# A fused attention and two-stage expert kernel: the end of attention and the first expert tiles in another order

## The reference

```python
# 1. gated linear attention, B=4, H=8, S=768, D=48
f = 1 / (1 + exp(-f_logit))
state = f[t] * state + outer(k[t], v[t]);  y[t] = q[t] @ state
# 2. top-1 experts: 3072 tokens, width 384, 8 experts, hidden 1024
logits = x @ w_gate + modality_bias[modality_id]
e = argmax(logits);  gate = softmax(logits)[e]      # denominator + 1e-9
x = gate * (relu(x @ w1[e]) @ w2[e])
# 3. gated MLP, hidden 1536
xn = x / sqrt(mean(x * x) + 1e-6) * rms_g
g = xn @ w_gate2
out = (g * sigmoid(g) * (xn @ w_val)) @ w_out
```

## Time and profile before

| | |
|---|---|
| median of 3 runs (lowest to highest) | 866.95 us (866.81 to 869.07) |
| profiled execution | 866.84 us, span 865.1 us |
| granted TensorE clock, mean | 0.988 |
| TensorE busy | 833.0 us, 96% |
| TensorE weight load | 762.5 us, 88% |
| VectorE busy | 471.8 us, 55% |
| ScalarE busy | 389.6 us, 45% |
| GpSimd busy | 165.6 us, 19% |
| DMA | 96.49 MB, mean 112 GB/s |

### The profile page before, as it was taken

The page is one execution under the profiler, slowest core; times in us unless marked ns, Lnnn a source line. Parts: engine busy times, 40 slices in busy tenths (PEclk is TensorE's granted clock), DMA queues, the critical chain, the costliest instruction groups (busy, mean ns, idle before and its releaser), DMA issues.

```text
span 865.1 us, 15457 instructions
## 1 busy us (share of the span) xinstructions
PE 833.0 (96%) x5332; PEld 762.5 (88%) x5332; DVE 471.8 (55%) x773; ACT 389.6 (45%) x750; POOL 165.6 (19%) x165
## 2 busy tenths in 40 slices
PE   6999999779999999989999999999999999999997
PEld 6798988779999999989888888888888898888887
DVE  7989898687766666653444333334333333433332
ACT  5988786375666555653423411331241133123112
POOL 5444352318554000000000200100020010001001
PEclk9999999889999999999999999999999999999999
DMA  9877666497988797750200200100020000000000
GB/s 182 188 148 169 150 146 210 153 387 239 301 258 260 245 344 255 255 147 20 74 1 1 74 0 1 66 8 0 0 73 0 0 28 8 0 0 36 0 0 36
DMA packets 44082, 96.49 MB, mean 112 GB/s; under 512 B 9168, under 2 KB 25040, under 8 KB 43920
## 3 DMA queue, kind: packets, MB, share of 16 engines
q1 hardware_dynamic: 39952, 85.81, 33.6%
q0 software_dynamic: 3840, 9.47, 3.1%
q10 hardware_dynamic: 256, 0.79, 0.4%
HBM read 76.75 MB, written 19.29 MB: 111 GB/s over the span
## 4 chain that ended last, share of the span: by engine, by line
PE 78%; issue 2%; DVE 1%; POOL 0%; ACT 0%; DVEq 0%; ACTq 0%
PE h_ps L1779 16%; PE h_ps L1781 15%; PE h_ps L1780 15%; PE ym_ps L1779 7%; PE ym_ps L1781 7%; PE ym_ps L1780 7%; PE xTm_ps L1780 3%; PE xTm_ps L1779 3%; PE xTm_ps L1781 3%; PE xT_ps L1796 1%; PE xTm_ps L1787 1%; POOL out L1443 0%; DVE h_lo L1691 0%; DVE w_lo L1664 0%; ACT w_hi L1461 0%
## 5 line engine op out<-in xcount | busy, mean ns | idle before, releaser
L1754 DVE TENSOR_TENSOR gs<-h_ps,sig 128x512 f32<-128x512 f32 x72 | 49.8, 691 | 175.5 <-ACT sig L1555 175.5
L1555 ACT ACTIVATE sig<-h_ps 128x512 f32<-128x512 f32 x72 | 43.1, 598 | 158.9 <-PE h_ps L1781 158.9
L1566 ACT CAST h_hi<-hid 128x512 fp32r<-128x512 f32 x72 | 44.6, 620 | 150.2 <-DVE hid L1757 150.2
L1779 PE MATMUL h_ps<-x_hi,w_hi 128*128 128x256 f32 x312 | 89.7, 287 | 7.7 <-DVEq L1682 5.1
L1781 PE MATMUL h_ps<-x_lo,w_hi 128*128 128x256 f32 x312 | 89.3, 286 | 0.0
L1780 PE MATMUL h_ps<-x_hi,w_lo 128*128 128x256 f32 x312 | 89.1, 285 | 0.0
L1779 PE MATMUL h_ps<-w_hi,wg_hi 128*128 128x512 f32 x216 | 85.5, 396 | 0.0
L1781 PE MATMUL h_ps<-w_lo,wg_hi 128*128 128x512 f32 x216 | 84.6, 392 | 0.0
L1781 PE MATMUL h_ps<-w_lo,wv_hi 128*128 128x512 f32 x216 | 84.2, 390 | 0.0
L1780 PE MATMUL h_ps<-w_hi,wv_lo 128*128 128x512 f32 x216 | 84.0, 389 | 0.0
L1779 PE MATMUL h_ps<-w_hi,wv_hi 128*128 128x512 f32 x216 | 84.0, 389 | 0.0
(11 more groups left out here) (222 smaller groups left out, 1890.0 us busy)
## 6 DMA issues: line engine op xcount, KB each, us to landing
w_raw<-in_w SPq DMA_DIRECT2D x52, 384.0 KB, 5.0
w_in<-in_w SPq DMA_DIRECT2D x52, 384.0 KB, 5.1
qkf_in<-in_qkf SPq DMA_DIRECT2D x43, 288.0 KB, 5.0
y_sorted<-x_group SPq DMA_DIRECT2D x13, 384.0 KB, 3.4
v_in<-in_v SPq DMA_DIRECT2D x24, 192.0 KB, 4.3
x_regions<-zero_row SPq DMA_DIRECT2D x12, 384.0 KB, 2.9
x_group<-x_regions SPq DMA_DIRECT2D x12, 384.0 KB, 3.9
g_in<-in_wg SPq DMA_DIRECT2D x3, 768.0 KB, 8.1
```

What stands on the lines that cost most here:

```text
L1555: nc.scalar.activation(sig[:], g_ps, ACT.Sigmoid).then_inc(sig_done, 1)
L1566: nc.scalar.copy(h2_hi[:, fb % HELD], hid[:]).then_inc(h2_hi_done, 1)
L1754: nc.vector.tensor_tensor(gs[:], g_ps, sig[:], ALU.mult).then_inc(gs_done, 1)
L1779: nc.tensor.matmul(out, hi, rhs_hi, start=first, stop=False)
```

## The change

It reorders; no arithmetic is added or left out.

1. Drain of attention: SP issues the weights of the first expert ahead of the last two v loads. Tile 23's keys are no longer transposed and copied (its state update is not used), and its read goes into the bank `ks_ps`, one phase earlier on TensorE, behind it the flag matmul and then the product of tile 22. ScalarE casts w1 quarters 0, 1, 2, 3 and copies in a new order. VectorE's flag steps, `lo_w1(2)` and `lo_x` move ahead of the logits of their step; `lo_w1(3)` moves into `experts`.
2. `experts`, tile 0: SP raises its semaphores ahead of three DMA issues, w2 first. ScalarE casts all four quarters of w2 at once. VectorE does `lo_w1(3)` behind `choose`. TensorE's count stands in the middle of hidden(0). `shifted_scores`, `rows_of_tokens`, `gates_of_tokens`, the Exp, the table load and thirds 0 and 1 leave the tile; `rows_of_tiles` goes to VectorE's end of it; `lo_w2(0, 3)` behind `lo_h(2)`. SP waits for rows_ready only before the store of y in tile 1.
3. Ends of middle tiles: VectorE does `shifted_scores` in tile 1, `rows_of_tokens` in tile 2, `gates_of_tokens` in tile 3. ScalarE casts third i in tile i + 1 (0 to 5 in tiles 1 to 6), with the Exp in tile 2. SP loads thirds 3 to 5 in tiles 3 to 5, `wo` in tile 8. POOL issues the token scatters eight at a time behind thirds 3, 4 and 5.
4. Last tile: ScalarE does `hi_h(0)` before the squares, and loads the sigmoid table behind `hi_h(1)`.

The diff, cut to its core:

```diff
@@ SP, attention
-            for b in range(2):
-                load_v(*tile(CH, b, 2))
-
             sp.wait_ge(ahead_sems.picked, PICKS)
             e = first.expert_of(sp)
             first.load_weights(sp, e, w1, w2, ahead_sems)
+            for b in range(2):
+                load_v(*tile(CH, b, 2))
@@ ScalarE, attention
-                if t := tile(c, b, 1):
+                if (t := tile(c, b, 1)) and not at(c, CH):
...
+                if at(c, CH) and b == 1:
+                    first.hi_w1(nc, act, 3, ahead_sems)
+                    kept(tile(c, b, 2), ks_ps)
...
                 if at(c, CH) and b == 0:
-                    first.hi_w1(nc, act, 1, ahead_sems)
+                    for g in range(2):
+                        first.hi_w1(nc, act, g, ahead_sems)
+                if (t := tile(c, b, 2)) and not (at(c, CH) and b == 1):
+                    kept(t, yT_ps)
+                if at(c, CH) and b == 0:
+                    first.hi_w1(nc, act, 2, ahead_sems)
...
+            def kept(t, acc):
+                _, s, n = t
+                act.wait_ge(y_done, n + 1)
+                wait_past(act, x_done, n - 1)
+                nc.scalar.copy(yT[:, s % 2], acc[:]).then_inc(yT_kept, 1)
@@ VectorE, attention
-                if at(c, CH) and b == 2:
+                if at(c, CH) and b == 1:
+                    first.lo_w1(nc, dve, 2, ahead_sems)
                     dve.wait_ge(flag_sum, 1)
...
+                if at(c, CH) and b == 2:
+                    first.lo_x(nc, dve, xT_ps, ahead_sems)
...
-                if at(c, CH) and b == 1:
-                    first.lo_w1(nc, dve, 2, ahead_sems)
-                if at(c, CH) and b == 2:
-                    first.lo_x(nc, dve, xT_ps, ahead_sems)
-                    first.lo_w1(nc, dve, 3, ahead_sems)
@@ TensorE, attention (read() is the old code of tile(c, b, 2))
-                    wait_past(pe, ks_done, n)
-                    for j in range(PR):
-                        mm = nc.tensor.transpose(ks_ps[:, j], kT[:, s, j], ident[:])
-                    mm.then_inc(k_turned, 1)
+                    if not at(c, CH):
+                        wait_past(pe, ks_done, n)
+                        for j in range(PR):
+                            mm = nc.tensor.transpose(ks_ps[:, j], kT[:, s, j], ident[:])
+                        mm.then_inc(k_turned, 1)
...
+                if at(c, CH) and b == 1:
+                    pe.wait_ge(ks_done, NT - 1)
+                    read(c, b, tile(c, b, 2), ks_ps)
+                    pe.wait_ge(small_ready, 1)
+                    nc.tensor.matmul(flag_ps, rt.ones_r[:], small[:], start=True, stop=True).then_inc(flag_sum, 1)
@@ experts
-        WO_AT = 7
+        WO_AT = 8
@@ SP, experts
+            sp.sem_inc(y_stored, 16)
+            sp.sem_inc(x_landed, 16)
+            for g in range(GR):
+                sp.sem_inc(w2_landed[g], 16)
+                sp.sem_inc(w1_landed[g], 16)
             for i in range(EARLY):
                 load_third(i)
...
                     load_third(EARLY)
-                    sp.wait_ge(rows_ready, 1)
...
                 if place == "middle":
+                    sp.wait_ge(rows_ready, 1)
                     store_y(j - 1)
...
-                            with only(sp, j, i - KD + 1):
+                            with only(sp, j, i):
                                 load_third(i)
@@ POOL, experts
-            pool.wait_ge(pos_ready, 1)
-            pool.wait_ge(gate_ready, 1)
...
-                for n in range(i * (NT // 6), (i + 1) * (NT // 6)):
+                if i == KD:
+                    pool.wait_ge(pos_ready, 1)
+                    pool.wait_ge(gate_ready, 1)
+                for n in range(max(i - KD, 0) * (NT // KD), max(i - KD + 1, 0) * (NT // KD)):
@@ ScalarE, experts
-            hi_w2(0, 0)
+            for g in range(GR):
+                hi_w2(0, g)
...
+                hi_h(0)
+                if place != "first":
+                    next_w1(0)
                 if place == "last":
                     act.wait_ge(norm_in, 16)
                     square(0, 0)
-                hi_h(0)
-                if place == "first":
-                    hi_w2(0, 1)
-                else:
-                    next_w1(0)
                 hi_h(1)
-                if place == "first":
-                    hi_w2(0, 2)
-                    act.wait_ge(shifted, 1)
-                    nc.scalar.activation(prob, biased, ACT.Exp).then_inc(exp_ready, 1)
+                if place == "last":
                     nc.scalar.preload_act_table_set("sigmoid_and_others")
-                    hi_w2(0, 3)
...
-                    hi_third(0)
...
-                if place == "first":
-                    hi_third(1)
                 if place == "middle":
-                    with act.If(j < 2 * KD):
-                        for i in range(EARLY, 2 * KD):
-                            with only(act, j, i - 1):
+                    with act.If(j < 2 * KD + 1):
+                        for i in range(2 * KD):
+                            with only(act, j, i + 1):
                                 hi_third(i)
+                                if i == 1:
+                                    act.wait_ge(shifted, 1)
+                                    nc.scalar.activation(prob, biased, ACT.Exp).then_inc(exp_ready, 1)
@@ VectorE, experts
-            dve.sem_inc(w1_split, GR)
+            dve.sem_inc(w1_split, GR - 1)
             dve.sem_inc(x_split, 1)
             rt.choose(nc, dve, CH - 1, marks, 0)
+            lo_w1(0, GR - 1)
             lo_w2(0, 0)
...
                     lo_w2(0, 1)
-                    shifted_scores()
                     lo_w2(0, 2)
-                    lo_w2(0, 3)
-                    rows_of_tiles()
...
                 lo_h(2)
                 if place == "first":
+                    lo_w2(0, 3)
...
                 if place == "first":
-                    rows_of_tokens()
-                    gates_of_tokens()
+                    rows_of_tiles()
+                if place == "middle":
+                    with dve.If(j < 4):
+                        with only(dve, j, 1):
+                            shifted_scores()
+                        with only(dve, j, 2):
+                            rows_of_tokens()
+                        with only(dve, j, 3):
+                            gates_of_tokens()
@@ TensorE, experts
                     for i in range(2):
+                        if place == "first" and g == 0 and i == 1:
+                            pe.wait_ge(marks, Routing.CHOSEN)
+                            rt.count(nc, pre_ps, cnt_ps).then_inc(counted, 1)
...
                 hidden(0)
-                if place == "first":
-                    pe.wait_ge(marks, Routing.CHOSEN)
-                    rt.count(nc, pre_ps, cnt_ps).then_inc(counted, 1)
                 hidden(1)
```

More of the change, by code:

```diff
@@ L722, in growth, with read @@
                 mm.then_inc(ds_done, 1)
+            def read(c, b, t, acc):
+                cc, s, n = t
+                if not tile(c, b, 1):
+                    pe.wait_ge(masked, n + 1)
+                if at(c, 0):
+                    pe.wait_ge(consts, CONSTS)
+                pe.wait_ge(v_landed[s], (cc + 1) * 16)
+                if not at(c, CH) and not (at(c, 0) and b == 2):
+                    growth(s, n)
+                wait_past(pe, state_done, n - 3)
+                if not at(cc, 0):
+                    for j in range(PR):
+                        nc.tensor.matmul(acc[:, j], state[:, s, j], qT[:, s, j], start=(j == 0), stop=False,
+                                         skip_group_check=True)
+                if at(cc, 0):
+                    pe.wait_ge(yT_zero, 1)
+                for j in range(PR):
+                    for par in range(2):
+                        h, r = 2 * j + par, PAD * par
+                        mm = nc.tensor.matmul(acc[r:r + D, j], v_in[:, s, D * h:D * (h + 1)],
+                                              scores[:, s % 2, par, j], start=at(cc, 0), stop=(at(cc, 0) or j == PR - 1),
+                                              skip_group_check=True)
+                mm.then_inc(y_done, 1)
             def step(c, b, half, more):
@@ L751, in step @@
                     mm.then_inc(x_done, 1)
[L752 to L772, removed]
-                            mm = nc.tensor.matmul(yT_ps[r:r + D, j], v_in[:, s, D * h:D * (h + 1)],
-                                                  scores[:, s % 2, par, j], start=at(cc, 0), stop=(at(cc, 0) or j == PR - 1),
-                                                  skip_group_check=True)
-                    mm.then_inc(y_done, 1)
+                if (t := tile(c, b, 2)) and not (at(c, CH) and b == 1):
+                    read(c, b, t, yT_ps)
                 if b == B - 1 and not (at(c, 0) or at(c, CH)):
@@ L782, in step @@
                 if at(c, CH) and b == 1:
-                    pe.wait_ge(small_ready, 1)
```

(8 more changed lines are left out.)

12 lines of the change are left out of this document (2 added, 10 removed).

## The result

The kernel after took 878.93 us (median of 4, 876.52 to 883.37) beside 868.01 of the kernel before (now the median of 4, the three of the table above and one of 873.08): a ratio of 1.012 with a 95% interval of 1.0062 to 1.0178. The forecast of 863.2 and its range up to 871.3 were both missed. The profiled execution took 878.87 us (span 877.1), 12.0 more than that of before.

What follows compares the result with a forecast made beforehand. TensorE, 96% busy, was taken as the bound, with some 13 us to be had at most. From 866.84 us, -6.95 - 0.32 + 0.3 + 3.3 = -3.65 gave 863.2 us, range 860 to 871.3.

Steps and rivals of the forecast that it cites:

- Into the experts, -0.75: Between attention and first expert tile: dropped transposes let POOL finish earlier, so TensorE starts at 159.55, 0.75 us sooner.
- Tile 0: First expert tile: table 1.05 us earlier, the 1.83 us wait goes, new wait about 2.4, clock +0.3 (0 to 0.65).
- Tile 1: Second expert tile: wait 1.3 instead of 3.17, half clock and 1.49 wait go; tile 2 starts at 202.3, -6.95 us.
- The ends of the tiles, +3.3: Ends of tiles 1, 2, 3: VectorE's moved chains make TensorE wait 0.9, 2.1 and 0.3 us, together +3.3 (1.8 to 12).
- 0.58 per chain: Ends of tiles 1 to 3: extra delay per chain beside POOL's subtractions, 0.73 - 0.15 us, from small ops.
- The row of 0.19: At 115.69 in the trace before: a small op inside a POOL operation of 1.51 us took its usual 0.19 us.
- The rival of the port: Ends of tiles 1 and 2: POOL's subtractions hold small VectorE ops, waits 3.3 and 5.1 us; 869.8 us, 27%.
- Eight token scatters per third instead of four: Middle tiles, POOL: the larger groups take some 10 us of a 17.67 us tile, cost nothing, covered by idle time.
- The last tile, -0.32: Last expert tile: squares follow h_hi(0), so the 0.32 us TensorE wait goes.
- chains hide entirely: Ends of tiles 1 to 3: rival in which the moved VectorE chains cost TensorE nothing; 861 us, 5%.
- one chain caught: End of tile 2: rival in which only its chain, longest under POOL, is held; +3 over forecast, 866.3 us, 15%.
- data bound: Tiles 0 and 1: rival in which data of tiles 1 and 2 land no earlier, the table's lead worthless; 865.5 us, 8%.

Runs made afterwards that it cites:

- b_scatter8: Kernel before with its token scatters grouped eight at a time behind thirds 3 to 5, nothing else touched: 873.89 us, ratio 1.005.
- the first trace: First profiled execution of the kernel after, unchanged: 878.87 us; median of that run 878.93 us, ratio 1.012.
- the first and the last experiments: First: four variants of the kernels, 869.29 to 875.69 us. Last, on a fourth chip: kernel after unchanged 881.07 us, and with a wait before each fourth scatter 871.25 us.
- b_scatter8_2: Kernel before with scatters in groups of eight, run again on a third chip: 866.99 us, ratio 0.9994.
- a_best_x: Version with both repairs, but SyncE loads tile 1's rows after the second instead of the fourth piece of w1: 863.59 us, ratio 0.995.
- a_best_x3: Version with both repairs, but SyncE loads tile 1's rows after the third instead of the fourth piece of w1: 863.01 us, ratio 0.9948.
- the version with both repairs: Kernel after with VectorE's chains in mid tile and scatters four at a time in tiles 5 to 10: 862.15 us (0.9941), repeated 864.27 us (0.9965).
- a_scatter4: Kernel after with its 24 token scatters four at a time over tiles 5 to 10, not eight over tiles 5 to 7: 873.01 us, ratio 1.0052.
- the first four experiments: Kernel after with scatters in fours, chains mid tile, or third casts later; kernel before with scatters in eights: ratios 1.0052, 1.0009, 1.0082, 1.005.
- after_fifth: Kernel after, unchanged, run again on a fourth chip: 881.07 us (two executions), ratio 1.0145.
- the third trace: Profiled execution of the kernel after, unchanged, run a third time, on a third chip: 869.79 us, ratio 1.0034.

## Why the prediction was wrong, point by point

- **Into the experts, -0.75: right in size, invisible in the time.** From the scores of the last but one step to the first expert matmul it was 160.30 - 142.08 = 18.22 us before and 160.31 - 142.70 = 17.61 after, 0.61 less; it is 17.60 to 17.69 in every trace with the new order, and 18.21 and 18.61 in the two of b_scatter8. All of it was lost in attention itself, whose end moves from run to run: in two traces of b_scatter8 the first expert matmul is at 158.80 and at 163.27.

```profile
142.70 1.22 DVE L631 TENSOR_TENSOR scores<-sc_ps,tri 128x1024 f32<-128x1024 f32 x1
```

- **Tile 0: the mechanism right, the clock too small.** The table was ready 9.66 us after the first expert matmul (169.97; forecast 9.75), and the rows were waited for 2.95 us (2.4). The clock behind that wait was counted at +0.3, up to 0.65. It was 0.66 in that stretch, and gather_y(3) with 12 matmuls took 185.46 - 181.73 = 3.73 us where a steady one takes 2.08: 1.6 us. Tile 1 started 25.15 us after the first expert matmul instead of 23.75.
- **Tile 1: right.** 18.67 us against 19.0, with a wait of 0.80 where 1.3 was forecast.
- **The ends of the tiles, +3.3: the step that failed.** Tile 1's chain cost 0.9, as said, tile 3's nothing, but tile 2's 7.2 instead of 2.1. The price of 0.58 per chain was taken from "a small op inside a POOL operation took 0.19" and another of 0.73, because they were nearest in size. Size did not spare them: operations that take 0.24 us alone took 1.36 and 1.20. The row of 0.19 was no measure of that, for it lies beside another form of GpSimd operation, with one source in place of two, and starts only 0.28 us before that ends. And the row of 0.73 (128.94 to 129.67) was a hold itself: a GpSimd operation that the forecast did not look up ends at 129.70. The two splits that were held lay beside the same subtractions as the new chains, and were the rows to take. The rival of the port priced tile 2's wait at 5.1 and had the sum at 869.8; where there was no stall, the kernel after measured 869.8 to 871.5. The cause is the rival's, but that its sum fits is in part luck: it had tile 1's chain at 3.3, which cost 0.9, while the gain up to tile 2 that it started from was 1.5 us too large. The mechanism differs in one point: three small operations were let in one by one, each as a subtraction ended, where the rival had the first held until the third ended. That is why tile 1's chain, of which a single operation was caught (1.39 us at 207.22), stayed cheap.

In the kernel before, GpSimd beside the earlier trace rows:

```profile
128.64 1.06 POOL L137 DMA_INDIRECT x_regions<-x_group,row  x1 [8.69 <-DVE row L132]
```

So the 0.58 was, as these rows have it, not the price of any collision but the rest of one GpSimd operation of 1.06; with three subtractions of 1.25 in a row the same reading gives three times up to 1.25. Which pairs of operations collide the runs show only in part: `chosen<-biased,first` (128x32, two sources, at 116.83) took 0.22 in the midst of a GpSimd DMA_INDIRECT of 1.06 (116.35).

- The Trainium skill's rule on this ("SBUF — State Buffer", section "SBUF: two separate sides"), that the shared pair of ports is locked for a whole instruction, agrees with the trace: 1.36, 1.20 and 1.36 us against subtractions of 1.25, and 0.24, 0.24 and 0.36 when GpSimd was away. The forecast set the row of 0.19 against it and left the rival at 27%; it deserved the larger share. What the runs show is the hold beside GpSimd's subtractions; that a port makes it is the page's account.
- **"Eight token scatters per third instead of four take some 10 us of a tile of 17.67; ... nothing, covered by idle time": the second step that failed.** GpSimd did have the time. What was not costed is what eight in a row do outside GpSimd: 7.2 us in tile 6 and 0.7 in tile 8, in the first trace, the like on the chips of the first and the last experiments, and nothing on the two others. No row of before showed more than four in a row, so the cost had no bound from above, and the forecast gave it none. Why the core stalls behind them stays open.
- **The last tile, -0.32:** 32.76 against 33.32 where the clock stayed up, -0.56. In the first trace the clock was 0.66 at its start and the tile 0.9 longer than before; the kernel before can have it too, for b_scatter8_2, whose last tile is the kernel before's, took 34.24.
- The rival "chains hide entirely" fell, and "one chain caught" had the right chain at 3 us over the forecast where it was 5.1; "data bound" did not decide the change, but it stopped a_best_x and a_best_x3.

## What to carry to other kernels

Work moved into idle time of one engine has to be asked twice: which engine shares a port with it there, and how many transfers it has under way. Price a collision from rows with the same neighbour, not from rows of the same size; and where a change raises a count above any that the trace shows, such as scatters in a row, give it an upper bound or spread it. The same change, with its chains some 7 us earlier and its scatters in fours, is 0.3 to 0.6% faster than the kernel before, measured on the two chips without the stall, where the change as it stood was 0.2 to 0.5% slower (with the stall 1.2 and 1.45%). On a chip with the stall the version with both repairs was not run; there scatters in fours took the stall away in a_scatter4.

## What the runs showed of the hardware that was not expected

- One program shows a stall of nearly the whole core on some chips (in the first trace, in those of the three kernels with eight in a row among the first four experiments, and in after_fifth: 23.8 to 25.0 us for a tile of 17.6) and none on two others. TensorE halts in mid group, with no wait in the code, and the DMA all but halts with it: the stretch from 282 to 287 moved 172 GB/s, and within it 284 to 286 moved 48 GB/s, while 79% of the DMA engines' time was busy; the third trace moved 390 GB/s in the same two microseconds. What halts them was not found. Each chip that stalled was met on one occasion only, so whether it is the chip or something else of that occasion is not shown.

```profile
282.00:287.00 5.00, 4.41 (x33) 4.05 (x32) 1.76 (x3) 1.64 (x4) 1.63 (x2) 1.00 0.79 172
```

- A wait of TensorE can cost more than itself: 2.95 us cost 1.6 more at the lower clock, 1.90 cost 1.7, and 4.96 cost about 2.2, while those of 0.70 and 0.80 left the granted clock at 1.00.
- VectorE's TENSOR_SCALAR with one large source and a column of scalars was held like those with two sources (1.36 us), while h_lo, which reads h_ps, took its 0.69 us in the midst of the subtractions of the earlier trace rows.
